# Two expert layers behind a recurrence: how tokens are routed, sorted and fetched

## The reference

```python
# 1. recurrence, B=4, H=8, S=768 steps, D=40 (state is 40 x 40 per batch and head)
y[:, :, t] = einsum('bhd,bhde->bhe', rt, state)
Sa = einsum('bhde,bhe->bhd', state, at)
state = state * wt - Sa (x) bt + vt (x) kt
x = y as [3072 tokens, 320]
# 2. expert layer 0 (E=8 experts, F=1024), one expert per token
logits = x @ w_gate;  e = argmax(logits);  gate = softmax(logits)[e] * sigmoid((x @ w_output_gate)[e])
out[i] = gate[i] * relu(x[i] @ w1[e]) @ w2[e]
# 3. expert layer 1: the same with other weights, no sigmoid, and a capacity:
#    an expert takes its first 768 tokens, a later token's output is 0
```

## Time and profile before

| stretch of the span, us | what it is | length |
|---|---|---|
| 0 to 576 | recurrence | 576 |
| 576 to 606 | logits of layer 0 | 30 |
| 606 to 619 | DVE's routing chain | 13 |
| 619 to 656 | scatter, first rows loaded | 37 |
| 656 to 955 | 31 expert tiles of layer 0 | 299 |
| 955 to 1000 | last store, reload, logits of layer 1 | 45 |
| 1000 to 1015 | routing chain | 15 |
| 1015 to 1051 | scatter, first rows loaded | 36 |
| 1051 to 1362 | 31 expert tiles of layer 1 | 311 |
| 1362 to 1374.7 | last results stored | 12 |

### The profile page before, as it was taken

One profiled execution on the slowest core, in us unless ns is written; L12 is line 12 of the kernel. 1 busy time (PEld: TensorE's weight loads), 2 busy tenths in 40 slices (PEclk: granted clock), 3 DMA queues, 4 the chain that ended last, 5 costly groups with the idle time before them and its releaser, 6 DMA issues.

```text
span 1374.7 us, 45515 instructions
## 1 busy us (share of the span) xinstructions
PE 1078.7 (78%) x19760; PEld 915.2 (67%) x19761; DVE 456.7 (33%) x867; ACT 286.8 (21%) x548; POOL 408.1 (30%) x350
## 2 busy tenths in 40 slices
PE   2278778878878888760899999997713999997996
PEld 1277767777777777520788888886303888886884
DVE  7554334544444330150223233231240232322321
ACT  0144333444443434310010110110100110100100
POOL 4453344433545412107022222121033122111211
PEclk9577687886887877885899999999856999999998
DMA  2344443534444211223133333332412313344110
GB/s 81 89 106 113 130 110 82 132 109 119 128 108 108 63 51 31 63 92 115 30 111 108 106 105 109 111 109 54 146 51 80 104 39 109 112 133 148 33 28 1
DMA packets 158725, 125.76 MB, mean 91 GB/s; under 512 B 91498, under 2 KB 136046, under 8 KB 158576
## 3 DMA queue, kind: packets, MB, share of 16 engines
q1 hardware_dynamic: 139216, 93.53, 24.6%
q10 hardware_dynamic: 12096, 14.09, 3.5%
q0 software_dynamic: 7264, 15.86, 3.3%
HBM read 89.57 MB, written 36.16 MB: 91 GB/s over the span
## 4 chain that ended last, share of the span: by engine, by line
PE 71%; POOL 8%; issue 6%; DVE 5%; DMA 4%; ACT 4%; SPq 1%; POOLq 0%; ACTq 0%; DVEq 0%
PE pair L1193 18%; PE pair L1174 16%; PE pair L1181 5%; POOL x_sorted L615 4%; POOL rvm L567 3%; PE bank L1045 3%; PE pair L1136 2%; PE pair L860 2%; PE pair L1026 2%; PE pair L1161 2%; PE bank L1052 2%; PE bank L956 2%; PE pair L925 2%; PE pair L894 2%; PE pair L911 2%
## 5 line engine op out<-in xcount | busy, mean ns | idle before, releaser
L1193 PE MATMUL pair<-abk_in,H_nat 128*128 x992 | 279.3, 434 | 1.7 <-DVE y_T L1446 1.7
L1174 PEld LDWEIGHTS pair<-y_T,rvm 128*128 128x128 f32 x1984 | 239.4, 198 | 20.9 <-issue 8.4
L1174 PE MATMUL pair<-y_T,rvm 128*128 128x128 f32 x1984 | 240.7, 281 | 9.8 <-DVE rvm L1431 7.4
L1193 PEld LDWEIGHTS pair<-abk_in,H_nat 128*128 128x128 f32 x992 | 183.5, 190 | 73.1 <-issue 3.0
L807 ACT ACTIVATE H_nat<-pair 128x512 f32<-128x512 f32 x62 | 37.0, 597 | 529.8 <-PE pair L1181 529.8
L1431 DVE COPY rvm<-AG 128x2560 f32 x62 | 95.2, 1536 | 100.9 <-issue 79.3
L567 POOL TENSOR_SCALAR_AFFINE_SELECT rvm<-rvm 64x1024 f32<-64x1024 f32 x48 | 79.0, 1646 | 112.6 <-ACT rvm L656 110.9
L1161 PE MATMUL pair<-table_sb,y_T 128*128 128x128 f32 x186 | 34.6, 296 | 92.5 <-DMA y_T<-x_sorted 92.5
L629 POOL DMA_INDIRECT out<-y_T,token_i x31 | 42.6, 1375 | 171.8 <-DVE y_T L1446 160.8
L1438 DVE TENSOR_SCALAR H_nat<-pair 128x512 f32<-128x512 f32 x62 | 42.7, 689 | 148.4 <-PE pair L1181 148.3
L553 POOL TENSOR_TENSOR AG<-abk_in,F_run 40x512 f32<-40x512 f32 x48 | 60.5, 1260 | 103.3 <-DVE T_nat L1275 84.0
(11 more groups left out here) (141 smaller groups left out, 1547.8 us busy)
## 6 DMA issues: line engine op xcount, KB each, us to landing
abk_in<-w SPq DMA_DIRECT2D x16, 1280.0 KB
y_T<-x_sorted ACTq DMA_DIRECT2D x62, 160.0 KB, 2.2
AG<-w SPq DMA_DIRECT2D x16, 512.0 KB
AG<-w SPq DMA_DIRECT2D x32, 256.0 KB
x_sorted<-empty SPq DMA_DIRECT2D x6, 1288.0 KB, 8.1
t_dram<-T_rows SPq DMA_DIRECT2D x12, 384.0 KB, 2.7
AG<-w SPq DMA_DIRECT2D x32, 128.0 KB
w_in<-wT SPq DMA_DIRECT2D x48, 80.0 KB
```

What stands on the lines that cost most here:

```text
L1174: mm(to, w1_now[:, par, k * F + m * P:k * F + m * P + P], xT[:, (0, 2 - m // 4)[k], :], start=(m % 4 == 0 and k == 0), stop=False, skip_gr ...
L1193: last = mm(bank[5][:, 0:DM], hidT[par][:, k, :], ring2[:, bass.ds(place, 1), k, :].rearrange("p a d -> p (a d)"), start=(k == 0), stop=(k ...
```

## The change

1. **First logits in the output's turn.** `turn_y`'s transposes become real products with `turns`, a matrix of 104 columns that holds the identity and, in the unused columns 40 to 55, the router's weights of layer 0 for these channels. `x_out` gets a third copy, of the partial logits, into `lg_parts`; one DVE reduction adds them up. x goes to `x_stage` and by SP to a DRAM buffer `x_dram` instead of `x_all`.
2. **Positions inverted by PE.** Instead of scattering rows, DVE builds two comparison matrices from each token's position, and 24 accumulated PE products turn them round: for each row of each tile the token's number and gate, kept in SBUF (`token_all`, `gate_all`).
3. **Rows gathered per tile.** POOL fetches the rows of a tile by an indirect read from `x_dram` or `between`; there are two buffers for rows and two for results. The blanking of `x_sorted`, the scatter, `load_rows`, `load_meta` and `tokens_of` are gone.
4. **Next logits per tile.** In layer 0 DVE multiplies each result tile by the next router's eight weight vectors (`wr_next`) and adds up; the eight logits travel with the row to `between`. Layer 1 loads only these, by one POOL DMA of 3072 pieces of 32 bytes.
5. **Early weights.** The first two experts' weights are loaded in the last slot but one of the recurrence, into a buffer of their own.
6. The tile loops are written out instead of looped; a few DVE steps of the chain are merged (eight running sums become one with restarts).

The core of the diff:

```diff
             def turn_y(k):
+                pe.wait_ge(router_in, 32)
-                        last = nc.tensor.transpose(pair[2][:, b, a * P:(a + 1) * P], y_T[:, b, a, :], ident)
+                        last = mm(pair[2][:, b, a * P:a * P + SPAN], y_T[:, b, a, :], turns[:, a, :],
+                                  start=True, stop=True)
...
             def x_out(k):
+                copy(lg_parts[:, 2 * s * NT + t:(2 * s + 1) * NT + t + 1:NT],
+                     pair[2][:, :, :].rearrange("p b (a t) -> p b a t", t=P)[:, :, :, D:D + 2 * E], x_copied)
...
         # SP, in the slots
-                if 0 <= j < 2 * CLEAR_PARTS:
-                    clear_sorted(j)
+                if j == -1:
+                    load_routers()
+                if j >= 2:
+                    sp.wait_ge(x_copied, 3 * (j - 1))
+                    write_x(j - 2)
+                if j == PREFETCH:
+                    sp.wait_ge(nat_ready, NU)
+                    sp.wait_ge(gk_ready, NU)
+                    for e in range(2):
+                        load_expert(0, e)
...
         # POOL
+                if s == 1:
+                    for n in range(2):
+                        pool.wait_ge(o_stored[0][n], 16 * tiles_by(MT, n))
+                    pool.dma_start(lg_all[:, :, 0:E], between[:, DM:ROW].rearrange("(t p) e -> p t e", p=P)
+                                   ).then_inc(lg_landed, 16)
                 pool.wait_ge(L["routed"][s], 1)
+                def gather(i):
+                    if i >= 2:
+                        pool.wait_ge(L["xt_ready"][s], i - 1)
                     pool.indirect_dma_start(
-                        out=x_sorted[s],
-                        out_offset=bass.IndirectOffsetOnAxis(ap=slot_i[:, t:t + 1], axis=0),
-                        in_=x_all[:, t, :], in_offset=None).then_inc(L["scattered"][s], 16)
+                        out=x_rows[i % 2][:, 0:(DM, ROW)[s]], out_offset=None, in_=source_of[s],
+                        in_offset=bass.IndirectOffsetOnAxis(ap=token_all[:, s, i:i + 1], axis=0),
+                        bounds_check=last_token, oob_is_err=False).then_inc(x_landed[s][i % 2], 16)
                 def send(i):
                     pool.wait_ge(L["o_copied"][s], i + 1)
+                    if s == 0:
+                        pool.wait_ge(lg_made, i + 1)
...
+                gather(0)
+                gather(1)
+                for i in range(MT):
+                    if i + 2 < MT:
+                        gather(i + 2)
                     send(i)
-                    load_meta(at)
...
         # PE, after the counts
+                for g in range(NG):
+                    if g % (NG // PARTS) == 0:
+                        pe.wait_ge(L["place_set"][s], g // (NG // PARTS) + 1)
+                    last = mm(bank[6][:, 0:2 * MT], in_place[:, g, :],
+                              carried[:, g, :, :].rearrange("p n m -> p (n m)"),
+                              start=(g == 0), stop=(g == NG - 1))
...
         # DVE: the start of layer 0's chain
+                    dve.wait_ge(x_copied, 3 * NK)
+                    link(v.tensor_reduce(lg_all[:, :, :], lg_parts[:, :, :, :].rearrange("p g a x -> p g x a"),
+                                         AX_X, ALU.add))
...
+                link(v.tensor_copy(place_i[:, :], best[:, :]))
+                link(v.tensor_scalar(row_i[:, :], place_i[:, :], P - 1, None, ALU.bitwise_and))
+                link(v.tensor_scalar(place_i[:, :], place_i[:, :], 7, None, ALU.logical_shift_right))
+                # in_tile [24 x 31], carried (two of [24 x 31]), then in four parts:
+                    v.tensor_tensor(in_place[:, n * lot:(n + 1) * lot, :], ...  # 6 x 128 each
...
+                def next_logits(i):
+                    dve.wait_ge(L["o_copied"][s], i + 1)
+                    if i:
+                        dve.wait_ge(lg_made, i)
+                    v.tensor_tensor(terms, wr_next[:, :, :],
+                                    y_rows[i % 2][:, 0:DM].unsqueeze(1).to_broadcast([P, E, DM]), ALU.mult
+                                    ).then_inc(terms_made, 1)
+                    dve.wait_ge(terms_made, i + 1)
+                    v.tensor_reduce(y_rows[i % 2][:, DM:ROW], terms, AX_X, ALU.add).then_inc(lg_made, 1)
...
+                for i in range(MT):
+                    if i + 2 < MT:
+                        stage_w1(i + 2, i % 2)
+                    if i + 1 < MT:
+                        relu1(i + 1, (i + 1) % 2)
                     result(i)
+                    if s == 0:
+                        next_logits(i)
```

More of the change, by code:

```diff
@@ L50 @@
 DM = H * D
-ROW = DM + 2
 NO_TOKEN = 4096
-LOT = 4
+PARTS = 4
 E = 8
+ROW = DM + E
 F = 1024
@@ L79 @@
     "eyes": D,
+    "turns": NPAIR * SPAN,
     "solve_init": BLK * BLK,
@@ L98, in tables @@
     t["eyes"][64 + d, d] = 1
+    for at in range(NPAIR):
+        t["turns"][d, at * SPAN + d] = 1
+        t["turns"][64 + d, at * SPAN + 64 + d] = 1
     j, i = np.arange(P)[:, None], np.arange(P)[None, :]
@@ L188, in recurrence_and_experts @@
         y_T = sb("y_T", [P, 2, NPAIR, P])
-        x_all = sb("x_all", [P, NG, ROW])
-        wr = [sb(f"router{s}", [P, 3, 2 * E]) for s in range(2)]
+        x_stage = sb("x_stage", [P, 2, 2, DM])
+        lg_all = sb("lg_all", [P, NG, 2 * E])
+        lg_parts = sb("lg_parts", [P, NG, NPAIR, 2 * E])
         cap_i = sb("cap_i", [P, 2], I32)
@@ L614, in _ @@
[L614 to L623 removed]
+                    for n in range(2):
+                        pool.wait_ge(x_written[n], 32 * NK // 2)
@@ L634, in send @@
[L634 to L648 removed]
+                        out_offset=bass.IndirectOffsetOnAxis(ap=token_all[:, s, i:i + 1], axis=0),
@@ L1167, in up @@
                     pe.wait_ge(L["w1_ready"][s], i + 1)
-                    if not (isinstance(i, int) and i < 2):
+                    if i >= 2:
                         pe.wait_ge(L["h_relu_act"][s], i - 1)
@@ L1200, in _ @@
                 turn_x(1)
-                def tile(i, par, up_next=True, turn_next=True):
-                    if up_next:
-                        up(i + 1, 1 - par)
-                    if turn_next:
+                for i in range(MT):
+                    if i + 1 < MT:
+                        up(i + 1, (i + 1) % 2)
+                    if i + 2 < MT:
                         turn_x(i + 2)
-                    down(i, par)
-                tile(0, 0)
-                with pe.Fori(1, (MT - 1) // 2) as j:
-                    tile(j * 2 - 1, 1)
-                    tile(j * 2, 0)
-                tile(MT - 2, 1, True, False)
-                tile(MT - 1, 0, False, False)
+                    down(i, i % 2)
         @block.vector
```

394 lines of the change are left out of this document (164 added, 230 removed).

## The result

The changed kernel takes 1655.22 us (median of 4 runs, 1647.04 to 1667.85) against 1382.62 (4 runs beside them, 1374.29 to 1385.77): ratio 1.199, 95% interval 1.194 to 1.205. Slower, as forecast, by more than forecast (1616), inside the range. The profiled execution took 1656.34 us, its span is 1654.6.

| stage, cut at the same events in both traces | before | after | difference | forecast |
|---|---|---|---|---|
| start to the end of `turn_y` (recurrence) | 575.2 | 596.9 | +21.7 | +9 |
| to the chain's first common step | 30.6 | 3.8 | -26.9 | -27.7 |
| chain and inversion, to POOL's first row DMA, two layers | 27.9 | 51.3 | +23.4 | +18.8 |
| first row DMA to first row transpose, two layers | 72.6 | 6.5 | -66.1 | -66 |
| tiles of layer 0, to the last `down`'s end | 299.8 | 569.7 | +270 | +281 |

What follows compares the result with a forecast made beforehand. PE, busy 78%, was taken as the bound. The terms +9 - 27.7 + 9.4 - 33 + 281 - 23 + 9.4 - 33 + 41 - 1 gave +232 on 1376.3, so 1608, as a median 1616 us; range 1530 to 1690.

Steps and rivals of the forecast that it cites:

- The closed loop, layer 0: Layer 0 tiles: down(i+1) waits for gather(i+3), queued behind send(i), which needs down(i); period 19.5 us against 9.45, +281.
- the sign named later: Layer 0 tiles: POOL's send should start about 6.5 us after result starts.
- Rival 1: Layer 0 tiles: the loop turns but PE's clock does not fall; period 16.9, total 1543; chance 0.15.
- rival 2: Layer 0 tiles: PE stays at half clock for all of down and the transposes; period 21.7, total 1678; chance 0.18.
- Layer 1: Layer 1 tiles: same loop without DVE's two passes, down ending at 11.2 against 9.45, no clock lost; +41.
- the one on layer 1: Layer 1 tiles: starts of down should be 10.5 to 12 us apart.
- The recurrence: Recurrence: longer transposes and ACT's third copy +9; transposed router load 0 to +6, taken 0.
- The inversion: PE's 24 products, 48 instructions per layer: 8.6 us, between 5.6 all warm and 10 all cold.
- First logits: From the recurrence's end to the chain: only the third copy 0.3 and one reduction 1.8 us remain; saves 27.7.
- Scatter to gather: First row DMA to first transpose: gather lands in 3.2 us where 36.5 and 36.1 passed before; saves 33 per layer.
- Between the layers: Layer 0's last down to layer 1's chain: 21.5 us instead of 44.9, load of 3072 pieces taking 11; saves 23.
- Rival 3: Tiles: not slower, POOL runs ahead and gathered rows are there in time; 1294; chance 0.04.

Runs made afterwards that it cites:

- 1: Changed kernel with POOL issuing gather(i+3) ahead of send(i), three gathers before the loop: 1293.89 us, ratio 0.938 to the kernel before.
- 2: Changed kernel with PE doing down(i) before turn_x(i+2), POOL's list as it was: 1378.65 us, ratio 1.000 to the kernel before.
- 7: Changed kernel with the first of next_logits' two DVE passes done twice, same values: 1751.68 us, ratio 1.267 to the kernel before.
- 3: Changed kernel with unread PE products before turn_x(i+2), seven per tile in layer 0, one in layer 1: 1588.6 us, ratio 1.153 to the kernel before.
- 5: Changed kernel with relu1(i+1) ahead of stage_w1(i+2) in DVE's list, both layers: 1644.92 us, ratio 1.189 to the kernel before.
- 6: Changed kernel with relu1(i+1) ahead of stage_w1(i+2) in DVE's list for layer 1 alone: 1617.28 us, ratio 1.172 to the kernel before.
- Experiment 4: Changed kernel with the transposed router load moved behind the recurrence in SP's queue: 1649.3 us, ratio 1.196 to the kernel before.
- 10: Changed kernel with gather ahead of send, transposed router load behind the recurrence, and 12 unread products before PE's inversion: 1275.61 us, ratio 0.922.
- experiment 8: Changed kernel with gather(i+3) ahead of send(i) and next_logits' first DVE pass done twice: 1378.58 us, ratio 0.998 to the kernel before.
- 11: Changed kernel with gather ahead of send, transposed router load behind the recurrence, and 9 unread products before PE's inversion: 1274.59 us, ratio 0.923.

## Why the prediction was right, and where it was not

- **The closed loop, layer 0** (+281, measured +270): right in place, order and size. Moving either of two list entries opens it (1 and 2), and a DVE pass of 2.83 us added to it costs 2.92 per tile (7). Its steps against the row of one tile: result 0.55 and passes 2.83 and 2.82 as taken; from result's start to the send 7.05 us (7.05 in the sum too, 7.25 - 0.2, though 0.75 + 5.6 stands there as 6.45; the sign named later, "about 6.5 us", is not the sum's own number); send 1.51 (1.4); landing 2.97 (3.2), which was a bound from another DMA. The clock cost 1.9 per tile (3) for 2.6 taken, and the period without that loss is 17.3 (3) for 16.9 taken: two small errors that cancel in part, 19.14 for 19.5. Rival 1, no fall, fell: granted clock 0.77; rival 2, half clock through the whole of `down`, needed 8.6 us of it, and it took 5.8 in the tile shown; `turn_x` took 0.90 instead of 0.55.
- **Layer 1** (+41, measured +92): the loop is the one that was forecast, and two terms of its sum were mis-sized. Against the 11.2 us taken for every held step, the 28 steps are 56 us longer in all (the rest of the stage is 5 shorter than forecast).
  - "gather issued at 3.25, landed 6.45", taken alike for all tiles: in the six that meet a load of weights the rows land 5.8 to 8.0 us after the gather's issue, not 3.2. These six steps make +34. The prediction held these loads to be covered by the median of the store's landings.
  - "Idle under 2 us; the 0.84 before the last `down` left it at 4.57, so no clock is lost": this was read from one row. In 11 steps PE idled 1.3 to 1.5 us and `down` took 6.26. They make +22. The other 11 make nothing in sum.
  - The copy of weights, which I had set against the send in layer 0, starts 1.5 us after result in layer 1 and meets the gather, +0.9. That the rows still came when forecast is luck: in the tile shown the gather went out at 2.35 on the prediction's scale, not 3.25 (POOL began 0.3 us after DVE, not 0.8, and the send took 1.01, not 1.4), and 3.9 later is 6.27 for 6.45. Experiments 5 and 6 take the collision away, and with 0.9 less idling the cold `down` goes too: -45. What is left, +47, is near +41 only because 22 of the 28 steps are then shorter than 11.2 (9.8 to 10.9) and six much longer.
  - Of the signs that the prediction named, the one on layer 1 failed: its steps lie between 10.5 and 12 us in 11 of 28.
- **The recurrence** (+9, measured +22): "0 to +6, taken 0" for the transposed load. I had priced the pieces as transfer on 16 engines; what they cost was SP's time to issue what stood behind them, 11 + 10 us. Experiment 4 gives back 14.9 in its own profile and 14.0 on the mean of all. The taken +9 for copies and transposes stands against about 8.
- **The inversion** (8.6, measured 10.50 in each layer): all 48 instructions were cold, which was the upper end; warm ones would take 5.5 (10), the lower end.
- **First logits** (-27.7, measured -26.9): the reduction took 2.7 us, not 1.8. **Scatter to gather**: -66.1 for -66.
- **Between the layers** (-23, measured -29.3): the load of 3072 pieces landed 4.7 us after its issue, for 11 taken. POOL's issue was as taken (1.48 for 1.5); the transfer, counted at the mean time of a packet in SP's queue, was far too long.

```profile
1209.44 1.48 POOL L648 DMA_DIRECT2D lg_all<-between  x1 [1.95 <-DMA between<-S_nat,token_all]
1214.18 0.35 DVE L1322 TENSOR_REDUCE best<-lg_all 128x24 f32<-128x192 f32 x1 [8.44 <-DMA lg_all<-between]
```

POOL's 1.48 us for 3072 pieces is far from 24 times the 0.57 of `meta`'s 128. The Trainium skill ("DMA: Bandwidth & Descriptors", on the anatomy of one DMA), which the prediction had weighed and put aside, was the better guide here: the 2.2 us estimated from its fit are 2.5 too short, the 11 taken 6.3 too long.

- **Rival 3**, the gathers in time, is no forecast of this kernel, but its number (1294) is what the kernel of experiment 1 takes. Its place, the order of POOL's list, was the deciding one; that the number fits to the microsecond is luck, as the 90 us of savings in it were 79 to 86.

What stays open: no run took the loads of weights away from layer 1's gathers, so the six late tiles rest on the comparison with the others and with layer 0. Why idling of 1.3 to 1.5 us left `down` at 4.57 in six steps and not in eleven is not shown either. Nor is it why the recurrence with the moved load varies by 13 us over four profiles, or why the median of experiment 8's kernel lies 9 us above its profiled execution.

## What to carry to other kernels

When work is moved into the shadow of a pipeline, write down for each engine's list what stands behind the new wait, and follow it round until it meets itself: a prefetch that is queued behind the store of an older tile has no depth at all, however many buffers it has. Price a DMA with many small pieces also by what is queued behind it on the issuing engine. And where an estimate rests on a slack of a microsecond, look for the instruction of another engine that will fill it, for the large load that some tiles issue at that moment, and for PE's clock.

## What the runs showed of the hardware

- An indirect DMA on POOL that starts while DVE copies 2560 float32 from SBUF to SBUF ends 0.9 us after the copy: 1.02 us alone, 1.51, 1.91 and 2.11 by where the copy stood. One that starts up to 0.46 us before the copy is held too, and ends 0.12 us after it (in the kernel before, 705.22 + 1.98 against 705.58 + 1.50); one that starts 0.62 us or more before it took 1.0. The Trainium skill ("SBUF — State Buffer", "Who interferes with whom") has contention of DVE and GpSimd as an exclusive lock of a shared port pair, and the trace agrees in that the DMA is held to the copy's end and not slowed in proportion.
- A `tensor_tensor` of DVE with both inputs in SBUF holds such a DMA as well: 3.62 us in 15 of 15 cases (8), and 3.41 for layer 0's last send but one. The same section of the Trainium skill tells of a probe in which `tensor_tensor` did not stall a DMA; here it did, and the measurement decides. A `tensor_scalar` with its input in PSUM did not hold one (1.02 us), and a DMA that began 0.01 us before a `tensor_tensor` took 1.02.
- 5.8 to 8.0 us passed from the issue of a gather of 128 rows to its landing when a load of 2.6 MB had been issued 2.2 us before, against 2.8 when it had been issued 8.9 us before.
- PE's granted clock falls to the lower of its levels (1.2 instead of 2.4 GHz) after short idling that comes back in each tile. Idling of 0.4 to 0.8 us per tile left `down` at 4.57 (6). At 1.3 to 1.5 us it took 6.26 in eleven tiles of the changed kernel's layer 1 and 4.57 in six, so the last gap alone does not decide. 2.12 us before the inversion gave 9.35 instead of 5.57 (11).
